# A seven-product matrix scheme on one core: the second product is accumulated onto the first one's PSUM bank instead of being added by GpSimd

## The reference

```python
f = lb + (1 - lb) * sigmoid(f_logit);  h = f[:, t] * h + (1 - f)[:, t] * x[:, t]    # the scan, y[:, t] = h
x = relu(y @ w_in1) ** 2 @ w_out1                                                   # first layer
g = x @ w_in2;  out = where(g > 0, g, exp(min(g, 0)) - 1) @ w_out2                  # second layer
```

## Time and profile before

| what | value |
|---|---|
| median of 3 runs | 1965.73 us (1965.67 to 1966.25) |
| profiled execution: span from first to last instruction | 1963.6 us |
| TensorE matmul busy | 1957.7 us (100%), 8712 matmuls |
| VectorE / ScalarE busy | 1604.5 us (82%) / 1518.6 us (77%) |
| GpSimd busy | 643.5 us (33%) |
| DMA | 281.54 MB, mean 143 GB/s |

### The profile page before, as it was taken

The page is one execution under the profiler, slowest core; times in us unless marked ns, Lnnn a source line. Parts: engine busy times, 40 slices in busy tenths (PEclk is TensorE's granted clock), DMA queues, the critical chain, the costliest instruction groups (busy, mean ns, idle before and its releaser), DMA issues.

```text
span 1963.6 us, 27999 instructions
## 1 busy us (share of the span) xinstructions
PE 1957.7 (100%) x8712; PEld 1632.4 (83%) x8712; DVE 1604.5 (82%) x1806; ACT 1518.6 (77%) x1848; POOL 643.5 (33%) x534
## 2 busy tenths in 40 slices
PE   9999999999999999999999999999999999999999
PEld 7888888888888888888888888888888888888888
DVE  7878887888888788888888888888888887866887
ACT  8898877877778777777777877777787777767766
POOL 4666632323223232232322323223232232332311
PEclk9999999999999999999999999999999999999999
DMA  6677453444444445344444444534434443443453
GB/s 196 204 228 227 165 150 106 148 145 127 147 135 125 130 147 146 107 148 136 126 147 142 127 124 144 147 111 150 135 119 148 145 130 113 137 136 118 140 172 112
DMA packets 228679, 281.54 MB, mean 143 GB/s; under 512 B 153857, under 2 KB 164098, under 8 KB 228610
## 3 DMA queue, kind: packets, MB, share of 16 engines
q1 hardware_dynamic: 226688, 280.23, 46.4%
q10 hardware_dynamic: 1922, 0.46, 0.1%
HBM read 248.25 MB, written 32.37 MB: 143 GB/s over the span
## 4 chain that ended last, share of the span: by engine, by line
PE 100%; DVE 0%; DVEq 0%; issue 0%
PE acc L626 53%; PE ring L626 46%; PE ring L663 0%; PE ring L778 0%; PE acc L785 0%; PE acc L663 0%; PE ring L785 0%; DVE o_sb L1719 0%; PE ring L823 0%; DVEq L116 0%; DVE m_sb L1632 0%
## 5 line engine op out<-in xcount | busy, mean ns | idle before, releaser
L626 PE MATMUL acc<-hid_hi,wout 128*128 128x512 f32 (+1 forms) x3072 | 1149.9, 387 | 0.0
L626 PE MATMUL ring<-t_hi,s_w 128*128 128x512 f32 (+1 forms) x2672 | 1027.3, 387 | 0.0
L626 PEld LDWEIGHTS acc<-hid_hi,wout 128*128 128x128 f32 x3072 | 576.8, 188 | 113.4 <-DMA wout<-w_kept 0.2
L626 PE MATMUL acc<-hid_lo,wout 128*128 128x512 f32 (+1 forms) x1536 | 594.7, 387 | 0.0
L626 PEld LDWEIGHTS ring<-t_hi,s_w 128*128 128x128 f32 x2672 | 501.7, 188 | 99.5 <-ACT xb L1182 0.3
L1895 POOL TENSOR_TENSOR xb<-xb,m_sb 128x512 f32<-128x512 f32 (+1 forms) x184 | 236.3, 1284 | 971.4 <-DVE hid_lo L1530 971.4
L626 PE MATMUL ring<-t_lo,s_w 128*128 128x512 f32 (+1 forms) x1336 | 517.2, 387 | 0.0
L1174 ACT ACTIVATE m_sb<-ring 128x512 f32<-128x512 f32 (+1 forms) x184 | 109.2, 593 | 354.1 <-PE ring L626 345.4
L626 PEld LDWEIGHTS acc<-hid_lo,wout 128*128 128x128 f32 x1536 | 288.4, 188 | 56.6
L626 PEld LDWEIGHTS ring<-t_lo,s_w 128*128 128x128 f32 x1336 | 250.9, 188 | 49.6
L1530 DVE TENSOR_TENSOR hid_lo<-xa,hid_hi 128x1024 fp32r<-128x1024 f32 (+1 forms) x191 | 231.3, 1211 | 61.4 <-ACT hid_hi L1153 61.2
(11 more groups left out here) (146 smaller groups left out, 1761.0 us busy)
## 6 DMA issues: line engine op xcount, KB each, us to landing
s_w<-s_kept SPq DMA_DIRECT2D x184, 512.0 KB, 3.8
s_w<-s_kept SPq DMA_DIRECT2D x184, 384.0 KB, 4.0
wout<-w_kept SPq DMA_DIRECT2D x88, 512.0 KB, 4.3
out_dram<-o_sb SPq DMA_DIRECT2D x88, 128.0 KB, 3.6
f_raw<-in_f_logit_dram SPq DMA_DIRECT2D x168, 64.0 KB, 3.5
x_raw<-in_x_dram SPq DMA_DIRECT2D x168, 64.0 KB, 2.7
s_kept<-ee SPq DMA_DIRECT2D x16, 512.0 KB, 4.1
s_kept<-s_w SPq DMA_DIRECT2D x8, 512.0 KB, 4.0
```

The lines of the kernel that those rows point to most:

```text
L626: mm = nc.tensor.matmul(out_ap, lhs[a], rhs[b], start=start and t == 0, stop=stop and t == 2)
```

## The change

`m2` leaves the ring. It is computed as before, but its three matmuls run without the flag that starts a new sum, on the bank in which `m1` lies, so that the bank then holds m1 + m2. The order of products in a step becomes m1, m6, m2, m7, m5, m3, m4, and the ring has six places per step. `m2` must now wait until ScalarE has copied `m1` alone out of the bank (`m1_kept`), since `u2` still needs it alone. ScalarE reads the sum from the bank (`c11_of`, in layer 1 with the Relu at once, so that `relu_of_n0` there has only half a tile), and GpSimd's addition and `m2_kept` are gone.

```diff
-ORDER = ("m1", "m2", "m6", "m7", "m5", "m3", "m4")
+ORDER = ("m1", "m6", "m7", "m5", "m3", "m4")
+BANK_OF = {"m2": "m1"}
...
@@ TensorE, step @@
                 if cur is not None:
-                    inputs_in(t_lbb, 1, 2)
+                    pe.wait_ge(sums_loaded[cur.par()], loads_of(cur))
+                    inputs_in(t_ltb, 1, 2)
                     bank_free(u4_done, relu_n1)
-                    product("m2", cur).then_inc(m2_done, 1)
+                    product("m6", cur).then_inc(m6_done, 1)
...
-                    pe.wait_ge(sums_loaded[cur.par()], loads_of(cur))
-                    inputs_in(t_ltb, 1, 2)
-                    bank_free(c12_done, relu_n0)
-                    product("m6", cur).then_inc(m6_done, 1)
+                    inputs_in(t_lbb, 1, 2)
+                    pe.wait_ge(m1_kept, cur.s + 1)
+                    product("m2", cur, False).then_inc(m2_done, 1)
...
                     inputs_in(t_lta, 1, 2)
-                    bank_free(c21_done, relu_n0)
+                    bank_free(c12_done, relu_n0)
                     product("m7", cur).then_inc(m7_done, 1)
...
-                    pe.wait_ge(m1_kept, cur.s + 1)
+                    bank_free(c21_done, relu_n0)
                     product("m5", cur).then_inc(m5_done, 1)
...
-                    pe.wait_ge(m2_kept, cur.s + 1)
+                    pe.wait_ge(c11_done, cur.s + 1)
                     product("m3", cur).then_inc(m3_done, 1)
@@ ScalarE @@
+            def c11_of(pr):
+
+                N = pr.N
+                act.wait_ge(m2_done, pr.s + 1)
+                act.wait_ge(lo_n0, pr.g - 1)
+                nc.scalar.activation(xb[:, pr.par(), 0, 0:N], bank("m2", pr),
+                                     ACT.Relu if pr.layer == 1 else ACT.Copy).then_inc(c11_done, 1)
...
@@ GpSimd, step @@
-                pool.wait_ge(lo_n1, cur.g)
-                N = cur.N
-                t = xb[:, cur.par(), 0, 0:N]
-                pool.wait_ge(m1_kept, cur.s + 1)
-                pool.wait_ge(m2_kept, cur.s + 1)
-                nc.gpsimd.tensor_tensor(t, t, m1_sb[:, 0:N], ALU.add).then_inc(c11_done, 1)
-                if nxt is not None:
+                if nxt is not None and (2 if late else 1) <= p < (8 if late else 7):
+
+                    pool.wait_ge(lo_n1, cur.g)
```

More of the change, by code:

```diff
@@ L164, in gated_scan_two_ffn @@
         m1_kept = sem("m1_kept")
-        m2_kept = sem("m2_kept")
         u2_done = sem("u2_done")
@@ L330, in bank @@
         def bank(name, pr):
-            return ring[:, (len(ORDER) * pr.p + ORDER.index(name)) % RING, 0:pr.N]
+            return ring[:, (len(ORDER) * pr.p + ORDER.index(BANK_OF.get(name, name))) % RING, 0:pr.N]
         def pieces_of(i):
@@ L622, in _, with triple, product @@
         def _(pe):
-            def triple(out_ap, lhs, rhs, start, stop):
+            def triple(out_ap, lhs, rhs, start, stop, onto=False):
                 for t, (a, b) in enumerate(((1, 0), (0, 1), (0, 0))):
-                    mm = nc.tensor.matmul(out_ap, lhs[a], rhs[b], start=start and t == 0, stop=stop and t == 2)
+                    mm = nc.tensor.matmul(out_ap, lhs[a], rhs[b], start=start and t == 0, stop=stop and t == 2,
+                                          skip_group_check=onto)
                 return mm
-            def product(name, pr):
+            def product(name, pr, start=True):
                 v = pr.phase.order % 2 if isinstance(pr.phase.order, int) else (pr.layer == 1) * 1
                 return triple(bank(name, pr), [s_w[:, pr.par(), SI[name], h, :] for h in range(2)],
-                              [t[v][:, TI[name], 0:pr.N] for t in (t_hi, t_lo)], True, True)
+                              [t[v][:, TI[name], 0:pr.N] for t in (t_hi, t_lo)], start, True, not start)
             def loads_of(pr):
@@ L1120, in n1_of @@
                     nc.scalar.activation(e, e, ACT.Exp, scale=-1.0).then_inc(acted_n1, 1)
+            def c11_of(pr):
[4 more added lines that the diff above has]
+                                     ACT.Relu if pr.layer == 1 else ACT.Copy).then_inc(c11_done, 1)
             def relu_of_n0(pr):
                 N = pr.N
-                act.wait_ge(c11_done, pr.s + 1)
                 act.wait_ge(c21_done, pr.s + 1)
@@ L1128, in relu_of_n0 @@
                 if pr.layer == 1:
-                    nc.scalar.activation(t, t, ACT.Relu).then_inc(relu_n0, 1)
+                    nc.scalar.activation(t[:, 1], t[:, 1], ACT.Relu).then_inc(relu_n0, 1)
                 else:
+                    act.wait_ge(c11_done, pr.s + 1)
                     if not (known(pr.phase.i, 0) and pr.p == 0):
@@ L1172, in step @@
                     act.wait_ge(u2_done, s)
-                    act.wait_ge(c11_done, s)
                 nc.scalar.activation(m1_sb[:, 0:N], bank("m1", cur), ACT.Copy).then_inc(m1_kept, 1)
@@ L1179, in step @@
                     relu_of_n0(last)
-                act.wait_ge(m2_done, s + 1)
-                act.wait_ge(lo_n0, g - 1)
-                nc.scalar.activation(xb[:, cur.par(), 0, 0:N], bank("m2", cur), ACT.Copy).then_inc(m2_kept, 1)
+                c11_of(cur)
                 if not after_plain:
```

## The result

The changed kernel takes 1968.52 us (median of 21 runs, 1968.18 to 1970.31) against 1965.57 us (median of 21, 1965.35 to 1967.13), a ratio of 1.0017 with a 95% interval of 1.0011 to 1.0023: 3 us slower, within the 0.2% that the prediction called no change, and clear of noise all the same. The 21 runs of the changed kernel fall into two groups: 12 from 1968.18 to 1968.77, and 9 from 1969.52 to 1970.31. The kernel before has one group with a thin tail: 18 of its 21 runs lie within 0.5 us, the other three at 1966.25, 1966.59 and 1967.13. The record gives each run's mean granted clock too: 0.999 in all nine of the upper group and 1.000 in all twelve of the lower one.

What follows compares the result with a forecast made beforehand. TensorE's closed string of matmuls was taken to bound the kernel; late loads of 2.66 us in step 0 and 0.09 in step 2 add 2.75 to 1965.73, giving 1968.5 us, own range 1967.9 to 1969.1, 8-in-10 range 1967.0 to 1971.2.

Steps and rivals of the forecast that it cites:

- Bound: Whole kernel: TensorE's string of matmuls at a fixed 0.227 us pace bounds; other engines' late weight loads cost 0.3 us.
- What it removes is worth nothing: GpSimd's 184 additions of 1284 ns, 236.3 us, gain nothing while TensorE keeps its pace.
- Slot 5, step 0: Slot 5's load waits for ScalarE's copy of m1 and starts 2.77 us late; 0.11 hidden, 2.66 us lost.
- step 10: Slot 11's load there came 0.21 us late before the change: 0.10 lost, 0.11 hidden; the 0.10 stays.
- Step 2: Slot 5's load waits for the copy of m1, 0.20 us late, 0.09 us lost.
- All other steps nothing: Moved waits elsewhere cost nothing: 0.78 us to spare at slot 5 ordinarily, `t_ltb` 0.7 us early at slot 3.
- The sum: Whole kernel: 2.66 + 0.09 = +2.75 us on 1965.73, giving 1968.5 us; chance 0.77.
- Rival A: TensorE's clock falls in step 0's pause: +2.6 to +3.6 us more, 1971.1 to 1972.1 us; chance 0.11.
- Rivals B: The wait for the copy of m1 bites in ordinary steps, 0.1 us lost 184 times: 1984 us; chance 0.03.
- C: No stall in step 0, ScalarE earlier or the wait met another way: 1965.7 us; chance 0.06.
- D: GpSimd's missing accesses quicken TensorE's matmuls: 1961 us; chance 0.03.

Runs made afterwards that it cites:

- the second experiment: The kernel before with only one wait added, m6 at slot 5 also waiting for ScalarE's copy of m1: 1969.95 us (11 runs).
- the first: The changed kernel with step 0 alone in the order m1, m6, m7, m5, m2, m4, m3: 1965.79 us, ratio 1.0001.

## Why the prediction was right

**Bound.** Right: nothing but TensorE's pace counted. The run without additions and the one with the early copy both stay at the time of before.

**What it removes is worth nothing.** Right, with the price of 1284 ns times 184 fully off the chain.

**Slot 5, step 0: 2.66 us.** Measured 2.71. The load came 0.11 us after the copy's end, not 0.05, and of a late load 0.1 us was hidden as forecast from step 10. That the wait alone makes it is shown by the second experiment, that nothing else does by the first.

**Step 2: 0.09 us.** Measured 0.08, at the place named.

**All other steps nothing.** Right at slot 5 in each of the other 182 steps; the margin of 0.78 us was tested with a delay of 0.6. `t_ltb` had 1.5 us to spare where I expected 0.7, since the load came 2.9 us later than before (173.18 against 170.29) and GpSimd, which waits for VectorE's `hid_lo`, could start only 2.0 us later (170.36 against the addition's 168.34).

**The sum: 1968.5 us.** The lower group's twelve runs lie around 1968.4. The median of 1968.52 is that of the lower group by a narrow margin: with 11 of 21 executions in the upper one it would have been near 1969.5.

**Rival A** is where the prediction was off. "Against it: 2.4 us is less than the 3.4 that the end survived at the full clock" failed, because one observation of a fall after 3.4 us bounds nothing from below. The same end was 2.0 us in the profile with step 0 reordered and 4.5 us in the one without additions. By their times the clock fell in 9 of 23 executions of this kernel, and I gave it 0.11, so the median came out as forecast partly by luck. Its price was mis-sized too: 2.6 to 3.6 us from the program's start, measured 1.7, since the low level lasted 3.4 us here and not 5 to 7. That price rested on the pace of the first matmuls alone; the granted clock reads 1.00 in the stretches of the start-up, which the prediction doesn't say. With the right price this rival ends at 1970.1, +0.23%, so the case that I kept apart from "no change" in truth lies on its edge. Rivals B, C and D didn't occur; GpSimd's busy time came to 417 us against my 407: three groups of what is left take longer (the sums of `z_raw`, now line 1810, 1667 ns against 1289, and two of `t_lo` 1395 and 1392 against 1304 and 1316), which the run without additions, with 407.6 us, does not show. What lengthens them stays open.

The Trainium skill's sentence that an idle array goes back to half speed ("TensorE: Matmul & The Clock Gate", "What's actually happening") agrees with the granted clock of 0.50 behind the pause in the profiles where the clock fell. It says nothing of which executions fall: by it alone every one would have lost, and 12 of 21 did not.

## What to carry to other kernels

When one engine runs as a closed string, list for each moved wait the margin in every step, not in the typical one: 181 steps had 0.78 us or more to spare and one 0.17, and nearly the whole loss came from one step behind the start-up phase, where the other engine had a backlog. Sharing a bank between two products cost no matmul time here that could be seen; it costs the margin of the reader between them, and here one early copy gives it back. And price a pause of the matrix engine of this size (2.45 to 3.49 us in these runs) at its length plus about one chance in two of 1.7 us for the clock.

## What the runs showed of the hardware that I had not expected

- The granted clock falls after pauses well under the 3.4 us that the end of the trace suggests: by the times, at 2.45 us between matmul starts in about half of the executions, at 1.93 us in none of 11, at 4.74 in all of 6. From 2.45 to 3.49 us so few executions show no dependence of the share on the pause (6 of 11, 18 of 35, 7 of 11). The fall itself is seen in one profile at 2.86, two at 3.49 and one at 4.74 us, and in none at 2.45.
- The low level lasts 3.41 us in each of the three profiles in which the clock fell at a pause of 2.86 or 3.49 us, and 6.83 us in the one with 4.74. It can begin behind the pause, under running matmuls: in the profile of the wait alone the matmuls were back at 92.86, and the clock fell at 93.31.
- Of a weight load that comes late, about 0.1 us is hidden: 0.42 us from load to load in step 2, 0.19 more than usual, cost 0.08 us between matmuls.
- GpSimd's additions made VectorE's scans longer: 1288 ns with them and 841 without, for the same 44 instructions.
